# Attention and two expert layers on one core: the sixteen heads written out, the first head loaded once and in pieces, and half of the routing moved into heads 9 to 11

## The reference, cut to what matters

```python
def _attn_ref(q, k, v):                       # B, H, S, D = 2, 8, 1152, 64
    q_pool = q.reshape(B, H, S // 2, 2, D).mean(axis=3)
    scores = scale * np.matmul(q_pool, k.transpose(0, 1, 3, 2))
    attn = softmax(scores)                    # written out in the reference
    return np.matmul(attn, v)

def _moe_ref(x, w_gate, w1, w2, capacity):    # N, D, E, F = 1152, 512, 8, 1024; capacity 288
    logits = x @ w_gate
    expert_idx = np.argmax(logits, axis=1)
    for i in range(N):                        # slots are dealt out in the order of the rows
        e = expert_idx[i]
        if counts[e] < capacity:
            disp[e, counts[e]] = x[i]
            pos[i] = counts[e]; counts[e] += 1; keep[i] = True
    h = np.maximum(np.einsum('ecd,edf->ecf', disp, w1), 0.0)
    y = np.einsum('ecf,efd->ecd', h, w2)
    out[i] = gate_w[i] * y[expert_idx[i], pos[i]]     # where keep[i]

def _moe2_ref(x, w_gate, w1, w2):             # 8 rounds of row and column scaling, then all experts
    for e in range(E):
        out += P[:, e:e + 1] * (np.maximum(x @ w1[e], 0.0) @ w2[e])
```

## Time and profile before

| what | value |
| --- | --- |
| median of three runs | 1380.02 us (1377.36 to 1382.0) |
| the profiled execution | 1380.57 us |
| its span, first to last instruction | 1378.8 us |
| PE busy | 1312.7 us, 95% |
| DVE, ACT, POOL busy | 518.6, 502.2, 490.0 us |
| attention, first expert layer, second layer end at about | 301, 549, 1379 us |
| mean granted TensorE clock | 0.982 |

### The profile page before, as it was taken

The page is one execution under the profiler, slowest core; times in us unless marked ns, Lnnn a source line. Parts: engine busy times, 40 slices in busy tenths (PEclk is TensorE's granted clock), DMA queues, the critical chain, the costliest instruction groups (busy, mean ns, idle before and its releaser), DMA issues.

```text
span 1378.8 us, 22483 instructions
## 1 busy us (share of the span) xinstructions
PE 1312.7 (95%) x7812; PEld 1227.3 (89%) x7812; DVE 518.6 (38%) x1321; ACT 502.2 (36%) x1029; POOL 490.0 (36%) x406
## 2 busy tenths in 40 slices
PE   4999999966999999799999999999999999999999
PEld 3998989966999999689899999999999999999998
DVE  4998989971222222414512222221112111211221
ACT  3777777763455545211311312312212212213111
POOL 5465555429577767401401402302202202203200
PEclk9999999987999999799999999999999999999999
DMA  6733333127556664400200300200201101100001
GB/s 147 216 96 87 86 87 86 57 96 249 185 163 205 209 203 152 135 0 1 92 32 0 122 0 26 96 0 30 91 0 59 62 0 61 61 0 0 0 0 68
DMA packets 61080, 112.44 MB, mean 82 GB/s; under 512 B 5727, under 2 KB 15523, under 8 KB 61032
## 3 DMA queue, kind: packets, MB, share of 16 engines
q1 hardware_dynamic: 52936, 94.92, 23.0%
q10 hardware_dynamic: 6624, 12.39, 2.9%
q0 software_dynamic: 1472, 4.54, 1.0%
HBM read 97.86 MB, written 14.16 MB: 81 GB/s over the span
## 4 chain that ended last, share of the span: by engine, by line
PE 89%; ACT 3%; DVE 3%; issue 2%; DMA 2%; POOL 0%; SPq 0%; DVEq 0%; ACTq 0%; POOLq 0%
PE psum L1168 36%; PE psum L1181 29%; PE psum L1200 7%; PE psum L1036 5%; PE psum L1026 4%; PE psum L1051 4%; PE psum L1066 1%; ACT acts L517 1%; ACT small L524 1%; ACT raw L524 1%; PE psum L1213 1%; PE psum L1158 1%; DMA raw<-in_k_dram 1%; PE psum L1131 0%; DVE acts L727 0%
## 5 line engine op out<-in xcount | busy, mean ns | idle before, releaser
L1168 PE MATMUL psum<-acts,wsplit 128*128 128x384 f32 (+1 forms) x3072 | 518.9, 328 | 2.5 <-issue 1.5
L1168 PEld LDWEIGHTS psum<-acts,wsplit 128*128 128x128 f32 x3072 | 508.8, 190 | 5.1 <-issue 2.0
L1181 PE MATMUL psum<-wsplit,acts 128*128 128x512 f32 x1728 | 397.6, 390 | 0.0
L1181 PEld LDWEIGHTS psum<-wsplit,acts 128*128 128x128 f32 x1728 | 323.9, 188 | 66.1
L447 POOL TENSOR_TENSOR wsplit<-raw,wsplit 128x512 fp32r<-128x512 f32 x128 | 162.5, 1297 | 497.7 <-ACT wsplit L517 497.7
L621 ACT ACTIVATE acts<-psum 128x384 fp32r<-128x384 f32 (+1 forms) x256 | 120.7, 471 | 574.5 <-PE psum L1168 573.9
L866 DVE SCALAR_TENSOR_TENSOR acts<-psum,acts 128x384 fp32r<-128x384 f32 (+1 forms) x256 | 136.2, 532 | 376.9 <-ACT acts L621 376.6
L452 POOL TENSOR_TENSOR wsplit<-raw,wsplit 128x512 fp32r<-128x512 f32 x128 | 161.0, 1296 | 135.0 <-ACT wsplit L517 135.0
L517 ACT ACTIVATE wsplit<-raw 128x512 fp32r<-128x512 f32 (+1 forms) x259 | 155.5, 623 | 89.2 <-PE psum L1181 75.2
L998 DVE SCALAR_TENSOR_TENSOR x<-psum,pr,x 128x512 f32<-128x512 f32 x63 | 47.3, 752 | 293.5 <-PE psum L1181 293.5
L517 ACT ACTIVATE acts<-psum 128x384 fp32r<-128x384 f32 (+2 forms) x282 | 116.2, 457 | 82.6 <-PE psum L1036 50.6
(11 more groups left out here) (119 smaller groups left out, 721.4 us busy)
## 6 DMA issues: line engine op xcount, KB each, us to landing
raw<-in_moe_w_dram SPq DMA_DIRECT2D x64, 1024.0 KB, 5.1
raw<-in_k_dram SPq DMA_DIRECT2D x32, 288.0 KB, 5.7
small<-in_q_dram SPq DMA_DIRECT2D x30, 288.0 KB, 4.3
small<-in_v_dram SPq DMA_DIRECT2D x16, 288.0 KB, 5.6
slots_in<-zero SPq DMA_DIRECT2D x1, 4608.0 KB
small<-slots_in ACTq DMA_DIRECT2D x8, 576.0 KB, 4.7
slots_out<-small ACTq DMA_DIRECT2D x7, 576.0 KB, 6.9
out_dram<-x ACTq DMA_DIRECT2D x9, 256.0 KB, 2.5
```

What stands on the lines that cost most here:

```text
L1168: last = mm(psum[:, f % HBANKS, 0:w], w1s[a][:, c, f * P:(f + 1) * P], src[z][:, c, cols], start=(i == 0), stop=(i == 3 * DC - 1))
L1181: last = mm(psum[:, bank, :], hs[a][:, f, t0:t0 + P], w2s[z][:, f, :], start=(i == 0), stop=(i == 3 * FC - 1))
```

## The change

- The 16 heads are written out on every engine; the loops over heads are gone.
- The host lays k, q and the first gate down twice, so that one load of 128 partitions brings what two loads of 64 brought before. For head 0 only one copy is loaded, k in three chunks of 384 columns; its queries have a place of their own (in x), and DVE sums them in two pieces of 256 and 320 columns, not POOL. So the queries of head 1 need not wait for head 0's split.
- The split of the second gate (wgs, L830) moves from before head 0's first `move_scores` to the end of head 2.
- `choose(0)` and `place(0)` are cut in pieces and stand in heads 9, 10 and 11, and the scatter of the first half stands on POOL after `split_head(12)`. The key split of head 13 waits for those transfers.
- The slot number is made in fewer steps: PE adds the expert's base to the counts, the limit is looked up ahead of the counts (`slot_limit`), the index is written as an integer at once. Seven of the eight heads of the second half are summed ahead of time (part). `tmp` and the scaling of x come after the steps on which the one-hot waits.
- POOL makes no `lo_w1` before the second scatter.
- The first expert's rows are loaded in two pieces, 128 columns and 384, and `hidden` for f = 0 waits for the rows column block by column block.

```diff
-        def over_heads(eng, body):
-
-
-
-            assert G % 4 == 0
-            body(0, 0)
-            body(1, 1)
-            with eng.Fori(0, (G - 4) // 4) as four:
-                for i in range(4):
-                    body(4 * four + 2 + i, (2 + i) % 4)
-            body(G - 2, (G - 2) % 4)
-            body(G - 1, (G - 1) % 4)
-
-
+        def over_heads(body):
+            for g in range(G):
+                body(g, g % 4)
...
-            def load_keys(g, u):
-                if not (isinstance(g, int) and g < 2):
-                    sp.wait_ge(ks_done, 2 * (g - 2))
-                for a in (0, 1):
-                    sp.dma_start(kraw[u][a * DH:(a + 1) * DH, :], kg[g]).then_inc(k_loaded[u], 16)
+            def load_keys(g):
+                u = g % 2
+                if g == 0:
+                    for c in range(NC):
+                        cs_ = slice(c * CH, (c + 1) * CH)
+                        sp.dma_start(kraw[0][0:DH, cs_], kg[0, 0:DH, cs_]).then_inc(k0_loaded[c], 16)
+                    return
+                if g >= 2:
+                    sp.wait_ge(ks_done if g > 2 else k0_done, 2 * (g - 2) if g > 2 else NC)
+                sp.dma_start(kraw[u], kg[g]).then_inc(k_loaded[u], 16)
 
             def load_queries(g):
-                sp.wait_ge(qs_done, g)
-                for a in (0, 1):
-                    sp.dma_start(qraw[a * DH:(a + 1) * DH], qg[g]).then_inc(q_loaded, 16)
-
-            def load_values(g, u):
-                if not (isinstance(g, int) and g < 2):
+                if g > 1:
+                    sp.wait_ge(qs_done, g - 1)
+                sp.dma_start(qraw, qg[g]).then_inc(q_loaded, 16)
+
+            def load_values(g):
+                u = g % 2
+                if g >= 2:
                     sp.wait_ge(vs_done, 2 * (g - 1))
                 sp.dma_start(vraw[u], vg[g]).then_inc(v_loaded[u], 16)
 
-            def load_head(g, u):
-                load_keys(g, u)
+            def load_head(g):
+                load_keys(g)
                 load_queries(g)
-                load_values(g, u)
+                load_values(g)
...
-            load_keys(0, 0)
-            load_keys(1, 1)
-            load_values(0, 0)
-            load_values(1, 1)
-            load_queries(1)
+            load_keys(0)
+            load_head(1)
+            load_values(0)
             sp.dma_start(wgr[:, :, :], moe2_w_gate.rearrange("(c p) e -> p c e", p=P)).then_inc(wg_loaded, 16)
-            for half in (0, 1):
-                for b in range(B):
-                    sp.dma_start(gfold[half * DH:(half + 1) * DH, b * NH:(b + 1) * NH, DH:FD],
-                                 moe_w_gate.rearrange("(h d) e -> d h e", d=DH)).then_inc(gate_loaded, 16)
-            load_head(2, 0)
-            load_head(3, 1)
+            sp.dma_start(gfold[:, :, DH:FD], moe_w_gate.rearrange("p b h e -> p (b h) e")).then_inc(gate_loaded, 16)
+            load_head(2)
+            load_head(3)
...
-            sum_queries(0)
...
+                if g == SCATTER0 + 1:
+                    pool.wait_ge(scattered, 16 * QT)
...
-            pool.wait_ge(zeroed, 32)
-            scatter_rows(0)
-            for f in range(FC // 4):
-                lo_w1(0, f)
+            for g in range(1, G):
+                split_head(g)
+                if g == SCATTER0:
+                    pool.wait_ge(zeroed, 32)
+                    scatter_rows(0)
+            pool.wait_ge(v_loaded[1], 16 * (G // 2))
+            pool.wait_ge(pv_ready, 2 * (G - 2))
+            values_hi(G - 1, 1)
+            values_lo(G - 1, 1)
             scatter_rows(1)
-            for f in range(FC // 4, FC):
+            for f in range(FC):
...
+            act.dma_start(q0raw, qg[0, 0:DH]).then_inc(q0_loaded, 16)
+            act.wait_ge(k0_loaded[0], 16)
+            split_hi(ksp[0][0:DH, 0:CH], kraw[0][0:DH, 0:CH], k0_hi)
+            for i, cols in enumerate((slice(0, QA), slice(QA, Q))):
+                act.wait_ge(q0_summed, i + 1)
+                for a in (0, 1):
+                    split_hi(qs[0][0][a * DH:(a + 1) * DH, cols], q0raw[:, 0, cols], q0_hi)
+                if i == 0:
+                    for c in range(1, NC):
+                        act.wait_ge(k0_loaded[c], 16)
+                        split_hi(ksp[0][0:DH, c * CH:(c + 1) * CH], kraw[0][0:DH, c * CH:(c + 1) * CH], k0_hi)
...
+                if isinstance(e, int) and e == 0:
+                    for i, cols in enumerate((slice(0, P), slice(P, DM))):
+                        act.dma_start(drow[:, :, cols], slots_in[0:CAP, cols].rearrange("(t p) d -> p t d", p=SR))\
+                           .then_inc(d0_loaded[i], 16)
+                    return
...
+                    if g == CHOOSE0:
+                        if t == 0:
+                            add_heads(lg[:, tiles(0), :], 0, NH)
+                            best_expert(0)
+                        elif t == 1:
+                            mark_expert(0)
+                        elif t == 2:
+                            one_hot(0)
+                        elif t == 4:
+                            slot_limit(0)
+                    if g == PLACE0 and t == TURN:
+                        slot_number(0)
+                    if g == PLACE0 and t == QT - 1:
+                        scatter_index(0)
+                    if g == PLACE0 + 1 and t == 0:
+                        gather_index(0)
+                    if g == 2 and t == QT - 1:
...
+            def slot_number(b):
                 ts = tiles(b)
                 dve.wait_ge(pos_ready, b + 1)
-                counts = psum[:, pos_bank(b), 0:QT * E].rearrange("p (t e) -> p t e", e=E)
-                rstep(nc.vector.tensor_tensor(cnt[:, ts, :], counts, oh[:, ts, :], ALU.mult))
+                link(pos_read, b + 1,
+                     nc.vector.tensor_tensor(cnt[:, ts, :], counts_in(b).rearrange("p (t e) -> p t e", e=E),
+                                             oh[:, ts, :], ALU.mult))
                 rstep(nc.vector.tensor_reduce(pos[:, ts], cnt[:, ts, :], AXX, ALU.add))
-                rstep(nc.vector.tensor_tensor(cnt[:, ts, :], ebase[:, ts, :], oh[:, ts, :], ALU.mult))
-                rstep(nc.vector.tensor_reduce(base[:, ts], cnt[:, ts, :], AXX, ALU.add))
-                rstep(nc.vector.tensor_tensor(base[:, ts], base[:, ts], pos[:, ts], ALU.add))
-                rstep(nc.vector.tensor_scalar(drop[:, ts], pos[:, ts], float(CAP), None, ALU.is_ge))
-
-                rstep(nc.vector.scalar_tensor_tensor(keep[:, ts], drop[:, ts], float(E * CAP), base[:, ts],
+
+            def scatter_index(b):
+                ts = tiles(b)
+                rstep(nc.vector.tensor_tensor(drop[:, ts], pos[:, ts], base[:, ts], ALU.is_ge))
+                nc.vector.scalar_tensor_tensor(sidx[:, ts], drop[:, ts], float(E * CAP), pos[:, ts],
+                                               ALU.mult, ALU.add).then_inc(idx_done, 1)
...
+            dve.wait_ge(q0_loaded, 16)
+            for cols in (slice(0, QA), slice(QA, Q)):
+                nc.vector.tensor_tensor(q0raw[:, 0, cols], q0raw[:, 0, cols], q0raw[:, 1, cols],
+                                        ALU.add).then_inc(q0_summed, 1)
+            k0_lo(0)
+            q0_lo(0, slice(0, QA))
+            for c in range(1, NC):
+                k0_lo(c)
+            for c in range(NC):
+                move_scores(0, 0, 0, c)
+            q0_lo(1, slice(QA, Q))
+            for c in range(NC):
+                move_scores(0, 0, 1, c)
+            dve.wait_ge(consts, 16)
+            nc.vector.tensor_scalar(elim[:, :, :], ebase[:, :, :], float(CAP), None, ALU.add).then_inc(lim_ready, 1)
+            nc.vector.tensor_scalar(ebase16[:, :, :], ebase[:, 0:QT, :], 1.0 / P, None, ALU.mult).then_inc(lim_ready, 1)
+            over_heads(head)
...
+            scale_logits(G - 1)
+            dve.wait_ge(lgh_done, G)
+            rstep(nc.vector.tensor_tensor(lg[:, tiles(1), :], lgh[:, :, G - 1, :], part[:, :, :], ALU.add))
+            best_expert(1)
+            mark_expert(1)
+            one_hot(1)
+            scale_output(G - 1)
+            slot_limit(1)
+            slot_number(1)
+            scatter_index(1)
+            gather_index(1)
+            nc.vector.tensor_tensor(tmp[:, :, :], lg[:, :, :], wide(mx), ALU.subtract).then_inc(ex_in, 1)
...
+                counts, t0 = counts_in(b), b * QT
+                mm(counts, ones16[:, :], ebase16[:, :, :].rearrange("p t e -> p (t e)"), start=True, stop=False)
+                for t in range(t0):
+                    mm(counts, ones16[:, :], oh[:, t, :].unsqueeze(1).broadcast_to([P, QT, E]), start=False, stop=False)
                 pe.wait_ge(oh_done, b + 1)
-                bank, t0 = pos_bank(b), b * QT
-                mm(psum[:, bank, 0:QT * E], upper[:, :], oh[:, t0:t0 + QT, :].rearrange("p t e -> p (t e)"),
-                   start=True, stop=False)
-                for t in range(t0 + QT - 1):
-                    z = max(0, t + 1 - t0)
```

(13 more changed lines are left out.)

226 lines of the change are left out of this document (120 added, 106 removed).

## The result

The median of the changed kernel is **1364.24 us** (1363.06 to 1365.16, four runs) against 1379.54 us (1377.36 to 1382.0, four runs) of the kernel before: ratio 0.9888, 95% interval 0.9869 to 0.9907, so 15.3 us faster by the medians. Predicted were 1361.0 us and a range of 1355 to 1367. The profiled execution took 1365.16 us, its span 1363.4, both 15.4 less than before.

What follows compares the result with a forecast made beforehand. PE was busy for 95% of the span, so the chain of waits was read where PE is not its owner. Terms -9.5 - 4.8 + 1.0 - 0.9 - 3.7 - 1.3 - 0.4 = -19.6 on 1380.57 gave 1361.0 us, range 1355 to 1367.

Steps and rivals of the forecast that it cites:

- start, to x of head 0: Kernel start: first exponential at 10.2 in place of 20.92, -10.7 us, taken as -9.5 because of the limit operations.
- heads written out: Loop over heads: two turns of the loop vanish, 2.4 us each, -4.8 us in all.
- routing in heads 9 to 11: Moved routing steps on DVE can stand behind POOL's splits: bounds nothing to 4.5 us, taken as +1.0.
- head 15, to its logits: Head 15: `place(0)` no longer ahead of the last `p_lo`, where PE waited 0.87 us; -0.9 us.
- load to first product: First expert's rows in two pieces: first product 1.9 us after the landing in place of 3.18, -1.3 us.
- clock in the first 96 products: First expert: with the gap before its first product closed, PE's clock may rise sooner; -0.4 us, between 0 and -0.6.
- Does the rest of head 0 follow?: Head 1's split on POOL ends at 19.1 to 22.5, before 24.4; cost zero, 2 us of cover in the worst case.
- Rival 1: Head 1's split is late, so heads follow POOL, not ACT; the start gives only 5.2 us, result 1365; chance 0.13.
- no such gap: Straight code in heads 0, 1, 14, 15 and inside each round had run without the loop turn's gap of 2.37 us.
- Rival 2: Moved routing meets POOL's splits each time: +4.5 us in place of +1, result 1364.5; chance 0.16.
- splits held back: First expert's weight splits on POOL after the transfers: hidden, ready before PE wants them, w2 pieces covered by 3 us.
- following with no wait: Sign at attention's end: PE's last value products follow with no wait.

## Why the prediction held, and where its steps failed

Differences of the two profiled executions, before to after:

| term | predicted | measured |
| --- | --- | --- |
| start, to x of head 0 (53.74 to 44.34) | -9.5 | -9.4 |
| heads written out | -4.8 | -3.5 |
| head 3, POOL's late split | 0 | +0.6 |
| routing in heads 9 to 11 | +1.0 | +2.9 |
| scatter in POOL's list | 0 | 0 or 1.2 to 1.7; 1.7 here |
| head 15, to its logits | -0.9 | -1.9 |
| logits to scatter index | -3.7 | -3.9 |
| load to first product (7.44 to 5.57) | -1.3 | -1.9 |
| clock in the first 96 products | -0.4 | -1.35 |
| wait for the data of expert 1 | 0 | +1.55 |
| sum | -19.6 | -15.4 (terms: -15.2) |

The changed kernel's median lies 0.24 us above the forecast's own band (1357.5 to 1364) and inside the range. The steps that failed were worth more than that: 7.2 us of errors on one side and 2.8 on the other, which cancel in part.

**Held: the start.** The step that gave 10.2 for the first exponential is right (10.33), and so, roughly, is its reserve of 1.2 us for the two limit operations: at x of head 0 they cost 1.66, as the run with them on POOL shows. So is "Does the rest of head 0 follow?": head 1's split starts at 11.50. But I followed the consequence for one head only. The zeros had the same place in SP's list, 9.4 us nearer to the heads that need what is behind them; the step "cost zero, with 2 us of cover" should have been made for head 4 too. Rival 1 had the mechanism (heads following POOL), at the wrong head and with 0.6 us for 4.

**Sizes off: written-out heads.** The turns are worth 2.4 each, as read. That straight parts of before showed "no such gap" was true of a gap, not of 0.1 us a head. The Trainium skill (Runtime: NRT & Kernel Launch, Instruction fetch mechanics) says that sequential fetch runs ahead and a taken branch breaks it; the turns' 2.4 us agree, though no run shows that fetching is what they were spent on, and the 0.1 us of a written-out head is not explained.

**Failed: routing at +1.0.** The reason I gave for the lower end, scores two tiles ahead, does not carry. All routing steps together are 5.6 us of DVE time, and 2.9 showed, without the loss around the scatter. In the run with short steps at t = 1 it is 3.4 us of DVE time, and 1.7 showed. Taken apart by the `p_lo` operations, the 2.9 are 0.8 for the sums at t = 0, 0.5 for the one-hot, 0.45 for the limit, 0.25 with PE's counts and 0.8 for the index. Rival 2 priced the waits behind POOL. They exist (0.45, 1.11 and 1.01 us against 0.20, 0.19 and 0.17 for the same steps after head 15), and the limit and the index in other tiles cost 1.1 less. So its cause accounts for a good third of the 2.9 and not for its +4.5; the steps' own time and PE's counts are the rest. The run agrees with the section Who interferes with whom of SBUF — State Buffer in the Trainium skill: under POOL's weight split the two-input steps took 1.10 and 0.96 us, the reduce 0.20. The forecast time of rival 2, 1364.5, is close to the result by chance: 1.9 us more of routing explain less than half of the 4.4 by which the sum missed.

**Failed: the earlier start of expert 0's products, credited in full.** The rows' pieces and the clock were taken off the total as if nothing stood behind them; "splits held back" asked only when PE wants POOL's pieces, which was covered, as I said. I did not ask whether the data of expert 1 come sooner as well. They do not. SP goes on with its loads when all the rows have landed, 4.14 us after their issue (306.79) and 4.23 before the change (320.71), so the pieces do nothing for them, and ACT has the data of its fifth copy 14.3 to 15.9 us after that. PE came 1.9 us sooner by the pieces and 1.35 by the clock, and 1.55 of that went into the wait. The run with two early splits shows that POOL's later end is not what made those data late.

**Never asked: the scatter's surroundings.** That the transfers fit into POOL's list held. That around their end 1.2 to 1.7 us are lost in some executions stood in no term; its cause is open.

**Sizes off, in favour:** the rows' two pieces (the four waits by column count as well as the landing, 1.9 for 1.3 at the first product); head 15, where PE's last wait fell from 0.87 only to 0.56, now behind ACT, against "following with no wait", and the rest came from the tiles where `choose(0)` stood, with waits like this one of before:

```profile
286.79 0.52 PE L1036 MATMUL psum<-ident,small 128*128 128x128 f32 x3 [0.42 <-DVE acts L727]
```

and the clock: with the gap closed the 96 products lost 1.35 us in this execution, and 0.4 to 1.3 in the others of the table above.

## What to carry to other kernels

When a change makes a stage start earlier, walk every queue that feeds the next stages, not the first one only: a transfer that was hidden where it stood can hold the loads behind it. A "free" operation put into the list of an engine that serves the critical one cost about half of its own time here; price it by its duration, and that by what it will stand behind. Before crediting an engine's earlier start in full, ask whether the data of its next piece of work come earlier too. And before naming the cause of a wait, look at both of its ends: a shorter wait can mean that the data came sooner or that the engine came later.

## What was not expected of the hardware

- A transfer issue can hold its engine long behind a large one: SP stood 15.10 us at a transfer of 2 KB behind one of 4608 KB, and 5.82 us behind a third of it.
- Operations with a single input stand behind POOL as well: the limits' first one took 1.01 us while POOL worked (13.05) and 0.20 in a gap between POOL's operations (19.23 in the run with the gate split back).
- The same 96 products took 14.36 to 15.33 us after the same code, at a granted clock of 0.90 to 0.83.
- Written-out heads run 0.1 us slower (16.75 against 16.65) than the same heads inside a loop of four.
- The second layer took 814.7 to 815.1 us in nine executions and 813.3 to 813.7 in five, in programs that are the same there: 1.4 us that single traces can mislead by.
- Around the end of five indirect transfers the engines stood 1.2 to 1.7 us in five of eight executions, with signals that came late from engines long done; three showed nothing, on two other chips than four of the five. The cause is open.
